# An earlier weight load and an earlier subtraction at the hand-over between two expert layers

## The chip, the cores and the metric

The kernel runs on one core of one Trainium2 chip. The metric is the device time of one launch in microseconds (us). The engines are called as the profile calls them: PE (TensorE, matmuls), PEld (its weight loads), DVE (VectorE), ACT (ScalarE), POOL (GpSimd) and SP (the queue that issues most transfers). "SPq" and "POOLq" are the instruction queues of SP and POOL.

## The reference, cut to what matters

Three layers run one after the other over 7168 tokens of 192 values: a windowed sum with per-token weights, a mixture of 8 experts with two choices per token, and a second mixture with one choice per token. The change lies where the second mixture ends its routing and begins its expert work:

```python
def _moe2_ref(x, expert_emb, tau, w1, w2):
    xn = x / (np.linalg.norm(x, axis=-1, keepdims=True) + 1e-06)
    en = expert_emb / (np.linalg.norm(expert_emb, axis=-1, keepdims=True) + 1e-06)
    logits = xn @ en.T / tau
    expert_idx = np.argmax(logits, axis=1)
    logits_shift = logits - logits.max(-1, keepdims=True)
    probs = np.exp(logits_shift)
    probs /= probs.sum(-1, keepdims=True) + 1e-09
    gate_w = probs[np.arange(N), expert_idx]
    for e in range(E):
        mask = expert_idx == e
        h = np.maximum(x[mask] @ w1[e], 0.0)
        out[mask] = gate_w[mask, None] * (h @ w2[e])
```

## The kernel before, in words

**Tokens and blocks.** Each mixture (`m` = 0, then 1) sorts its tokens by expert into blocks of 256 slots. `positions(m)` on DVE computes each token's slot, turns the slots into one-hot rows (7 groups for m = 1, line 1256), ACT scales half of them by row codes (`hot_rows`, line 1028), and PE multiplies them (line 772) to obtain the list of token rows per slot. DVE then reads that list (`gather_rows`), and the expert work starts.

**Expert work.** `mixture(m)` exists once per engine. For each block `g`, PE computes two products in eight chunks `c` (lines 808 to 824). At chunk `c == TURN_AT` (2) of block g it transposes the token rows of block g+1 (`turn_slots`, lines 789 and 790), for which they must have been gathered: `pe.wait_ge(gathered[m], g * 32 + 64)`. PE takes its instructions in order, so a late gather stops everything behind it. POOL issues each gather as two indirect transfers of 128 rows (line 533), one per half block, from `gather_before(g)`, which fetches block g+3. It waits until PE has turned block g+2, since there is one buffer `x_slots`.

**Gates in the second mixture.** The gathered row of `token_rows[1]` has a last column for the token's gate. The gates are not ready when the first blocks of m = 1 are gathered; blocks 0 to 2 are gathered without them (their gates come by small separate gathers, line 541), and SP meanwhile writes the whole gate column into `token_rows[1]` (line 455, 7168 single values). From block 3 on the gather brings the gate, so `gather_before(0)` on POOL waits for that column: `pool.wait_ge(gate_column_in, 16)`.

**Expert weights.** SP loads each expert's weights (`load_expert`, line 381: four transfers of 512, 256, 256 and 768 KB into `raw1` and `raw2`). ACT and DVE split them into two parts (lines 972, 978, 1310 and 1314) during the first block of the expert before; each finished split raises `weights_ready`, after which `raw` may be overwritten. In m = 1, experts 0 and 1 are loaded before the routing; expert 2 and the later ones come in a loop of SP. That loop stands behind the write of the gate column and, before the change, behind the arrival of the fourth gather (block 3): `sp.wait_ge(gathered[1], 4 * 16 * HALVES)`.

**The subtraction.** The softmax of the second mixture needs each score minus the best one. DVE computes it in `below_best` (line 1372), which `positions(1, below_best)` calls behind the copy of the membership table (line 1204) and ahead of its own wait for PE's ranks (PE lines 758 and 759, then DVE line 1209). `step()` lets DVE wait for the instruction that it has just issued.

Of the kernel before, what the change touches and what calls it, by code (L numbers as in the profile page):

```python
# [16 lines left out]
P = 128  # L17
ALU = mybir.AluOpType
# [8 lines left out]
HALVES = BLOCK // P  # L27
# [24 lines left out]
def attention_moe_moe(nc, x, weight_gen, m_gate, m_noise, noise, w1, w2, emb, tau, v1, v2, w2t, out):  # L52
    B, S, D = x.shape
    H, K = weight_gen.shape[2:]
    E, _, F = w1.shape
    G = D // H
    J = S // P
    T = B * J
# [33 lines left out]
    with ExitStack() as ctx:  # L92
        def sb(name, shape, dt=F32, at=ctx):
            return at.enter_context(nc.sbuf_tensor(name, shape, dt))

        def sem(name):
            return ctx.enter_context(nc.semaphore(name))
# [53 lines left out]
        r = {n: sb(n, [P, T, E]) for n in ("noisy", "tie", "pos", "picked")}  # L151
        onehot = [sb(f"onehot{k}", [P, T, E]) for k in range(2)]
        best = [sb(f"best{k}", [P, T]) for k in range(2)]
# [116 lines left out]
        gate_column_in = sem("gate_column_in")  # L270
# [10 lines left out]
        gathered = [sem(f"gathered{m}") for m in range(2)]  # L281
# [93 lines left out]
        def _(sp):  # L375
# [76 lines left out]
            for b in range(B):  # L452
# [1 line left out]
            sp.wait_ge(gathered[1], 3 * 16 * HALVES)  # L454
            sp.dma_start(tile_rows(token_rows[1], 0, T)[:, :, DS:DS + 1], gate[0][:].unsqueeze(2),
                         allow_slow_non_contiguous=True).then_inc(gate_column_in, 16)
            sp.wait_ge(gathered[1], 4 * 16 * HALVES)

            with sp.Fori(2, E) as e:
                sp.wait_ge(weights_ready, e + E)  # L460
# [202 lines left out]
        def _(pe):  # L663
# [33 lines left out]
            def sum_products(g, inner=None):  # L697

                if g >= 2:
                    pe.wait_ge(rows_ready, g - 1)  # L700
                for n, (tap, _) in enumerate(PAIRS):
                    pe.wait_ge(taps_added, g * len(PAIRS) + n + 1)
                    for h in range(2):
                        ins = mm(banks[:, 2 * (g % 2) + h, 0:GHALF], ident[:], prods[g % 2][:, tap, h * GHALF:(h + 1) * GHALF],  # L704
                                 start=n == 0, stop=n == len(PAIRS) - 1)
                    if n == 1 and inner is not None:
                        inner()
                ins.then_inc(sums_done, 1)
# [159 lines left out]
        def _(act):  # L868
# [80 lines left out]
            def mixture(m, behind_first_split=None):  # L949
                def x_hi(g):  # L950

                    hi_a, _, part_b = x_buffers(parity(act, g))
                    act.wait_ge(x_turned[m], g + 1)
                    sc.copy(hi_a, banks[:, 3, 0:BLOCK])
                    sc.copy(part_b[0:DB], banks[0:DB, 3, BLOCK:]).then_inc(x_hi_ready[m], 1)
# [129 lines left out]
        def _(dve):  # L1085
            v = nc.vector
            steps = [0]

            def step(ins):

                steps[0] += 1
                ins.then_inc(dve_step, 1)
                dve.wait_ge(dve_step, steps[0])
# [49 lines left out]
            def pick(k, scores, at=slice(0, T)):  # L1143

                shape = [P, at.stop - at.start, E]
                tie, top = r["tie"][:, at, :], best[k][:, at]
                step(v.tensor_reduce(top, scores[:, at, :], AX.X, ALU.max))
                step(v.tensor_tensor(tie, scores[:, at, :], top.unsqueeze(2).to_broadcast(shape), ALU.is_equal))
                ranks = expert_rank[:].unsqueeze(1).to_broadcast(shape)
                step(v.tensor_tensor(tie, tie, ranks, ALU.mult))  # L1150
                step(v.tensor_reduce(rank[:, at], tie, AX.X, ALU.max))
                step(v.tensor_tensor(onehot[k][:, at, :], ranks, rank[:, at].unsqueeze(2).to_broadcast(shape), ALU.is_equal))
# [214 lines left out]
            scores = logits[:, :, 0:E]  # L1367
            dve.wait_ge(scores_in, 16)
            pick(0, scores)

            def below_best():
                step(v.tensor_tensor(r["noisy"][:], scores, best[0][:].unsqueeze(2).to_broadcast([P, T, E]), ALU.subtract))

            def weigh_best():
                dve.wait_ge(roots_ready, 1)
# [5 lines left out]
            def finish_best():  # L1381
# [2 lines left out]
                step(v.tensor_scalar(gate_sum[:], gate_sum[:], 1e-9, None, ALU.add))  # L1384
                v.reciprocal(gate[0][:], gate_sum[:]).then_inc(gates_ready[1], 1)

            positions(1, below_best)
            dve.wait_ge(x1_in[NG - 1], 16)
            last = slice((NG - 1) * GROUP, T)
            step(v.tensor_tensor(rows[:, last, :], rows[:, last, :], rows[:, last, :], ALU.mult))  # L1390
# [33 lines left out]
```

## Time and profile before

| What | Value |
|---|---|
| median of 3 runs | 1145.79 us (1145.06 to 1146.03) |
| profiled execution, its time | 1145.06 us |
| its span in the trace | 1143.2 us |
| PE busy | 1055.1 us (92% of the span) |
| DVE, ACT, POOL busy | 708.5, 532.3, 626.9 us |
| granted clock of PE, mean | 0.978 of full speed |

The span is the stretch from the first to the last instruction of the profile; the 1.9 us between it and the execution's time lie around it. Times in the rows further down are microseconds from the start of the span. The first mixture's expert work runs to about 776 us, the second's routing to about 819 us, and its expert work from there to the end.

### The profile page before, as it was taken

What the parts mean: (1) busy time and instruction counts of PE and PEld (TensorE: products, weight loads), DVE (VectorE), ACT (ScalarE), POOL (GpSimd) and SP (SyncE); (2) the same over time, 40 slices, a digit from 0 to 9 for tenths busy, and PEclk for the clock granted to TensorE, in tenths of its full rate; (3) what the DMA queues carried; (4) which work ended last, traced back from release to release, by engine and by line L of the source; (5) the groups of instructions that cost most, each with busy time, mean ns of one, the idle gap of its engine ahead of it and who ended that gap; (6) DMA issues with size and microseconds to landing.
All of it is one profiled execution on the core that took longest, in us unless ns stands there. A gap on an engine that the chain in (4) does not pass through costs nothing.

```text
span 1143.2 us, 27409 instructions
## 1 busy us (share of the span) xinstructions
PE 1055.1 (92%) x7707; PEld 990.4 (87%) x7707; DVE 708.5 (62%) x1474; ACT 532.3 (47%) x1471; POOL 626.9 (55%) x761
## 2 busy tenths in 40 slices
PE   1989988999999999999999999992699999999997
PEld 0556437999999999999999999991499999999997
DVE  8999884556565565555645656444846464567663
ACT  2122574445454454544544545443945454456553
POOL 6888103555565555555556555552265555555554
PEclk9999999999999999999999999996799999999999
DMA  9656995325335252252532524337362231133611
GB/s 333 182 160 166 290 72 131 51 39 105 42 50 98 42 105 41 42 106 41 106 45 39 105 41 83 63 39 143 97 94 74 73 105 42 42 101 99 169 36 35
DMA packets 121939, 106.50 MB, mean 93 GB/s; under 512 B 45971, under 2 KB 111818, under 8 KB 121628
## 3 DMA queue, kind: packets, MB, share of 16 engines
q1 hardware_dynamic: 92316, 69.10, 26.0%
q0 software_dynamic: 29568, 36.73, 18.8%
q8 instruction: 27, 0.44, 0.2%
q14 instruction: 28, 0.23, 0.1%
HBM read 70.61 MB, written 35.73 MB: 93 GB/s over the span
## 4 chain that ended last, share of the span: by engine, by line
PE 79%; DMA 6%; DVE 6%; POOL 3%; issue 2%; ACT 2%; DVEq 0%; SPq 0%; POOLq 0%; ACTq 0%
PE banks L822 23%; PE banks L824 11%; PE banks L808 8%; PE banks L814 7%; PE banks L813 7%; PE banks L809 7%; PE banks L810 7%; PE banks L704 3%; DMA x_slots<-token_rows,gather_idx 3%; DVE prods L1123 3%; POOL prods L521 2%; PE banks L789 2%; PE banks L790 2%; ACT hi_rows L1028 1%; ACT wide L1067 1%
## 5 line engine op out<-in xcount | busy, mean ns | idle before, releaser
L1339 DVE SCALAR_TENSOR_TENSOR h_lo<-banks,h_hi 128x256 fp32r<-128x256 f32 x736 | 312.0, 424 | 351.6 <-ACT h_hi L1009 346.6
L1009 ACT ACTIVATE h_hi<-banks 128x256 fp32r<-128x256 f32 x736 | 283.0, 384 | 433.3 <-PE banks L814 430.2
L822 PE MATMUL banks<-w_hl,h_hi 128*128 128x400 f32 (+1 forms) x1472 | 474.9, 358 | 1.2 <-DVE h_lo L1339 1.2
L824 PE MATMUL banks<-w_hl,h_lo 128*128 128x200 f32 (+1 forms) x1472 | 373.7, 254 | 0.0
L824 PEld LDWEIGHTS banks<-w_hl,h_lo 128*128 128x128 f32 x1472 | 280.3, 190 | 0.0
L822 PEld LDWEIGHTS banks<-w_hl,h_hi 128*128 128x128 f32 x1472 | 277.4, 188 | 1.6 <-issue 1.4
L533 POOL DMA_INDIRECT x_slots<-token_rows,gather_idx x188 | 188.6, 1003 | 112.4 <-POOL gather_idx L526 80.0
L576 POOL DMA_INDIRECT token_rows<-y_slots,store_idx x120 | 194.2, 1619 | 85.5 <-POOL store_idx L571 51.7
L808 PE MATMUL banks<-x_hi_a,w_hi 128*128 (+1 forms) x736 | 221.8, 301 | 1.7 <-DVE x_hl_b L1293 1.7
L810 PE MATMUL banks<-x_lo_a,w_hi 128*128 (+1 forms) x736 | 207.3, 282 | 0.0
L814 PE MATMUL banks<-x_hl_b,w_lo 128*128 (+1 forms) x736 | 207.2, 282 | 0.0
L813 PE MATMUL banks<-x_hl_b,w_hi 128*128 (+1 forms) x736 | 207.2, 282 | 0.0
L809 PE MATMUL banks<-x_hi_a,w_lo 128*128 (+1 forms) x736 | 207.0, 281 | 0.0
L808 PEld LDWEIGHTS banks<-x_hi_a,w_hi 128*128 128x128 f32 x736 | 138.4, 188 | 4.6 <-issue 3.2
L809 PEld LDWEIGHTS banks<-x_hi_a,w_lo 128*128 128x128 f32 x736 | 140.6, 191 | 0.0
L814 PEld LDWEIGHTS banks<-x_hl_b,w_lo 128*128 128x128 f32 x736 | 139.5, 190 | 0.0
L813 PEld LDWEIGHTS banks<-x_hl_b,w_hi 128*128 128x128 f32 x736 | 139.1, 189 | 0.0
L810 PEld LDWEIGHTS banks<-x_lo_a,w_hi 128*128 128x128 f32 x736 | 138.6, 188 | 0.0
L704 PE MATMUL banks<-prods,ident 128*128 128x384 f32 x168 | 67.3, 532 | 34.8 <-POOL prods L521 34.8
L529 POOL COPY gate_ring<-x_slots 128x2 f32 (+1 forms) x89 | 16.8, 189 | 143.8 <-PE banks L790 143.0
L578 POOL DMA_INDIRECT out_rows<-y_slots,store_idx x64 | 66.3, 1037 | 45.3 <-issue 42.0
L1123 DVE TENSOR_TENSOR prods<-x_halo,banks 128x3072 f32<-128x3072 f32 (+1 forms) x28 | 81.3, 2947 | 3.0 <-ACT banks L892 1.8
(194 smaller groups left out, 1133.9 us busy)
## 6 DMA issues: line engine op xcount, KB each, us to landing
raw<-in_moe_w SPq DMA_DIRECT2D x17, 768.0 KB
token_rows<-stage SPq DMA_DIRECT2D x28, 384.0 KB, 4.7
raw<-in_moe_w SPq DMA_DIRECT2D x17, 512.0 KB
raw<-in_moe_w SPq DMA_DIRECT2D x34, 256.0 KB
wide<-in_moe_w_turned SPq DMA_DIRECT2D x8, 768.0 KB, 12.2
token_rows<-zeros SPq DMA_DIRECT2D x14, 402.0 KB, 6.2
x_halo<-in_x SPq DMA_DIRECT2D x2, 2688.0 KB, 15.4
wide<-token_rows SPq DMA_DIRECT2D x14, 384.0 KB, 7.1
```

What stands on the lines that cost most here:

```text
L533: gp.indirect_dma_start(x_slots[:, i, 0:ROWS[m]], None, token_rows[m], bass.IndirectOffsetOnAxis(gather_idx[:, i:i + 1], 0)).then_inc(gath ...
L576: ins = gp.indirect_dma_start(token_rows[1], at, y_slots[:, u, i, :], None, compute_op=ALU.add)
L808: mm(to, w1_hi[u][:, 0, f], hi_a, start=True, stop=False)
L809: mm(to, w1_lo[u][:, 0, f], hi_a, start=False, stop=False)
L810: mm(to, w1_hi[u][:, 0, f], lo_a, start=False, stop=False)
L813: mm(to, w1_hi[u][:, 1, f], part_b, start=False, stop=False)
L814: mm(to, w1_lo[u][:, 1, f], part_b, start=False, stop=True).then_inc(h_done[m], 1)
L822: mm(y[:, i, 0:2 * WIDTH[m]], h_hi[:, c % HBUFS, t], w2_hl[u][:, c, :, 0:WIDTH[m]], start=c == 0, stop=False)
L824: ins = mm(y[:, i, 0:WIDTH[m]], h_lo[:, c % HBUFS, t], w2_hl[u][:, c, 0, 0:WIDTH[m]], start=False, stop=c == FC - 1)
L1009: sc.activation(h_hi[:, c % HBUFS, :], banks[:, c % HBANKS, 0:BLOCK], ACT.Relu).then_inc(h_hi_ready[m], 1)
L1123: v.tensor_tensor(prods[g % 2][:, at:at + n].rearrange("p k (a c) -> p k a c", c=G), x_taps, w_taps, ALU.mult).then_inc(done, 1)
L1339: v.scalar_tensor_tensor(h_lo[:, c % HBUFS, :], banks[:, c % HBANKS, 0:BLOCK], 0.0, h_hi[:, c % HBUFS, :].bitcast(F32), ALU.max, ALU.subtr ...
```

## The change

Two edits. SP's loop over the experts 2 to 7 of the second mixture waits for the gate column to have been written, and no longer for the gather of block 3 to have arrived. DVE subtracts the best score ahead of the membership copy, and no longer between that copy and the wait for the ranks; `positions(1)` is called without a function for that place.

```diff
             sp.wait_ge(gathered[1], 3 * 16 * HALVES)
             sp.dma_start(tile_rows(token_rows[1], 0, T)[:, :, DS:DS + 1], gate[0][:].unsqueeze(2),
                          allow_slow_non_contiguous=True).then_inc(gate_column_in, 16)
-            sp.wait_ge(gathered[1], 4 * 16 * HALVES)
+            sp.wait_ge(gate_column_in, 16)
 
             with sp.Fori(2, E) as e:
                 sp.wait_ge(weights_ready, e + E)
                 load_expert(v1, v2, e)
...
             pick(0, scores)
-
-            def below_best():
-                step(v.tensor_tensor(r["noisy"][:], scores, best[0][:].unsqueeze(2).to_broadcast([P, T, E]), ALU.subtract))
+            step(v.tensor_tensor(r["noisy"][:], scores, best[0][:].unsqueeze(2).to_broadcast([P, T, E]), ALU.subtract))
...
-            positions(1, below_best)
+            positions(1)
```

## Rows read from the trace of the kernel before

**Rows 1.** The page, the chain that ended last, shares by engine.

```profile
PE 79%; DMA 6%; DVE 6%; POOL 3%; issue 2%; ACT 2%; DVEq 0%; SPq 0%; POOLq 0%; ACTq 0%
```

**Rows 2.** Timeline of DVE: start, duration, line, operation, idle before and its releaser.

```profile
793.27 0.62 DVE L1152 TENSOR_TENSOR onehot<-expert_rank,rank 128x448 f32<-128x448 f32 x1
793.93 0.39 DVE L1204 CAST member<-onehot 128x448 bf16<-128x448 f32 x1
794.24 0.61 DVE L1372 TENSOR_TENSOR noisy<-logits,best 128x448 f32<-128x448 f32 x1
795.42 0.62 DVE L1209 COPY counts<-banks 128x448 f32<-128x448 f32 x1 [0.56 <-PE banks L759]
...
802.36 0.46 DVE L1256 TENSOR_TENSOR hots_hi<-column_no,slot_hl 128x576 bf16<-128x576 bf16 x1
...
808.19 0.45 DVE L1256 TENSOR_TENSOR hots_hi<-column_no,slot_hl 128x576 bf16<-128x576 bf16 x1
...
830.03 0.56 DVE L1314 TENSOR_TENSOR w_hl<-raw,w_hl 128x384 fp32r<-128x384 f32 x1
```

**Rows 3.** Timeline of ACT.

```profile
802.92 6.71 ACT L1028 ACTIVATE hi_rows<-hots_hi,row_code_i 128x288 bf16<-128x288 bf16 x14
...
871.30 0.61 ACT L972 CAST w_hi<-raw 128x512 fp32r<-128x512 f32 x1
```

**Rows 4.** The chain that ended last, from 828 us on: start, duration, what.

```profile
827.26 10.81 DMA token_rows<-gate
```

**Rows 5.** Timeline of SP: the first two weight loads of its loop.

```profile
843.34 2.31 SPq L381 DMA_DIRECT2D raw<-in_moe_w  x4
...
881.19 2.62 SPq L381 DMA_DIRECT2D raw<-in_moe_w  x4
```

**Rows 6.** Timeline of PE: turns of gathered rows ahead of which it stood idle.

```profile
177.25 0.30 PE L789 MATMUL banks<-ident,x_slots 128*128 128x128 f32 x1 [4.04 <-DMA x_slots<-token_rows,gather_idx]
...
843.06 0.33 PE L789 MATMUL banks<-ident,x_slots 128*128 128x128 f32 x1 [0.71 <-DMA x_slots<-token_rows,gather_idx]
...
853.54 0.33 PE L789 MATMUL banks<-ident,x_slots 128*128 128x128 f32 x1 [0.50 <-DMA x_slots<-token_rows,gather_idx]
```

**Rows 7.** Timeline of POOL: issues of indirect transfers, and one gate copy.

```profile
840.38 0.95 POOL L533 DMA_INDIRECT x_slots<-token_rows,gather_idx  x1 [0.30 <-issue]
...
845.22 0.99 POOL L578 DMA_INDIRECT out_rows<-y_slots,store_idx  x1 [0.30 <-issue]
...
847.14 0.19 POOL L529 COPY gate_ring<-x_slots 128x2 f32 x1 [0.49 <-POOL gate_ring L546]
...
849.64 0.97 POOL L533 DMA_INDIRECT x_slots<-token_rows,gather_idx  x1 [0.30 <-issue]
...
886.42 0.98 POOL L533 DMA_INDIRECT x_slots<-token_rows,gather_idx  x1 [0.31 <-issue]
```

**Rows 8.** DMA queues, 840 to 842.75 us: packets, MB, share of 16 engines.

```profile
q0 software_dynamic: 96, 0.21, 26.7%
```

**Rows 9.** DMA queues, 844.25 to 847 us.

```profile
q1 hardware_dynamic: 208, 0.77, 91.1%
q0 software_dynamic: 2, 0.01, 1.5%
```

**Rows 10.** DMA queues, 847 to 849.5 us.

```profile
q0 software_dynamic: 52, 0.11, 18.5%
```

**Rows 11.** DMA queues, 886.5 to 889 us.

```profile
q1 hardware_dynamic: 812, 0.65, 104.7%
q0 software_dynamic: 1, 0.00, 0.6%
```

**Rows 12.** DMA queues, 889 to 892 us.

```profile
q0 software_dynamic: 143, 0.30, 31.6%
```

**Rows 13.** Windows: length, busy PE, PEld, DVE, ACT, POOL, granted clock, DMA, GB/s.

```profile
178.00:180.00 2.00, 2.00 (x6) 0.57 (x4) 0.84 (x2) 1.12 (x3) 1.13 (x3) 0.50 0.02 2
180.00:182.00 2.00, 2.00 (x14) 2.00 (x15) 0.35 (x1) 0.77 (x2) 1.09 (x2) 0.75 0.50 66
```

## The prediction

> **What bounds the kernel now.** I read the page first: the chain that ended last is PE for 79% [rows 1]. In the expert work of the second mixture PE runs without gaps, so that a microsecond by which PE stands longer there is a microsecond of the kernel. I then asked for the chain, the waits and the timelines around the place of each edit. The reader should see three things there.
>
> First, the routing. The chain runs from the scores over DVE and ACT to PE. DVE makes the one-hot groups and ACT scales each of them as it comes.
>
> Second, the gate column. Its write takes 10.81 us, from 827.26 to 838.07 [rows 4], and it is on the chain: POOL may gather block 3 only behind it. The second half of that gather is issued from 840.38 to 841.33 [rows 7], PE turns the block at 843.06, and has stood idle for 0.71 us by then [rows 6]. There is thus no slack at all in the gather of block 3.
>
> Third, the weight load of expert 2. SP issues it at 843.34 [rows 5], right behind the arrival of that gather. It is not this load's own data that anybody waits for, neither before nor after the change, as shown below. What matters is which gathers it shares the DMA engines with.
>
> **The subtraction (DVE).** Nothing is added or removed, one instruction of 0.61 us moves. Where it stands now it is free: DVE ends it at 794.85 and stays idle for another 0.56 us until PE's ranks release the copy at 795.42 [rows 2]. Where it goes, it lies ahead of the membership copy, and PE's ranks, the counts and everything behind them wait for that copy. Its price there is its pitch with the step's wait, read at its neighbour of the same shape: 793.27 to 793.93, 0.66 us, call it 0.65. The idle gap behind the copy grows from 0.56 to what it takes without the subtraction, and pays nothing back.
>
> Could ACT hide it? ACT squares the rows of the first eight groups before it turns to the one-hot groups, and starts those at 802.92; the first group has been ready since 802.36 + 0.46 = 802.82. At the last of the seven groups DVE is ready at 808.19 + 0.45 = 808.64, and ACT, whose 14 instructions end at 802.92 + 6.71 = 809.63, that is 0.96 a group, starts it at about 808.67 [rows 2, 3]. So ACT lags by 0.10 us at first and by 0.03 at the end: of 0.65 us it hides 0.03. The term is **+0.6 us** (bounds 0.55 and 0.66). Behind it the list of rows, the gathers, the gates and the column all shift by as much.
>
> **SP's wait.** The new wait ends when the column has landed, 838.07 + 0.6 = 838.7. The other wait of the loop, for the split of expert 1, ends with the last DVE part at 830.03 + 0.56 = 830.6 [rows 2], and is no cover. From the arrival of what released it to its first issue SP took about 0.3 us before (843.06 to 843.34). The load is then issued from 839.0, 4.9 us before its shifted old place of 843.9. In SP's queue only the later loads of the loop stand behind it, and each of those waits for a split of its own.
>
> What does the earlier load bring? Nothing: ACT reads expert 2's `raw` first at 871.30 [rows 3], some 20 us after the load is through. It has a cost, since POOL issues the gather of block 3 at the same moment: its second half from 841.0 to 841.9, 2 to 3 us behind the start of a load of 1792 KB.
>
> **How late does a gather come that shares the engines with such a load?** Alone, the whole gather is 96 packets, all served by 842.75 [rows 8], 1.4 us behind the end of its second issue; PE moves 1.7 us behind that end. With a load there are three places to read:
>
> (a) The gather of block 4. Its second issue ends at 850.61 and PE moves at 853.54 [rows 6, 7]: 2.9 us instead of 1.7, so 1.2 us late. It meets only the tail of its load, having been issued 7.3 us behind the load's start.
>
> (b) The second load, issued at 881.19 [rows 5]. The gather beside it has its second issue done at 887.40 [rows 7]. From 886.5 to 889 the software queue q0, which serves POOL's transfers, moves 1 packet while q1 moves 812 [rows 11]; then 143 packets pass from 889 to 892 [rows 12]. If they end at 892, that is 4.6 us behind the issue instead of 1.4: 3.2 us late. PE does not stand idle for it there, since it comes to that block later; behind 853.54 no such stop is left in the expert work.
>
> (c) The nearest in position: POOL's two stores of block 0. The second is issued from 845.22 to 846.21 [rows 7], 1.9 to 2.9 us behind the load of 843.34, just where the second half of block 3's gather will stand. In 844.25 to 847 q0 moves 2 packets beside 208 of q1 [rows 9], 52 in the next 2.5 us [rows 10]. So the first store is through at about 849 and the second at about 851, some 7.7 us behind the load's start. A gather in its place is through at 839.0 + 7.7 = 846.7, instead of 842.75 + 0.6 = 843.4: 3.3 us late.
>
> I take **+3.2 us**, by (b) and (c), because they lie in the body of a load, as the new gather does. The bounds: nothing, if the gather's packets slip in before the load has filled the engines (its first half is issued 1.3 us ahead of its second, hardly a microsecond behind the load); and at the far end (b) taken whole, 892 less 881.19 = 10.8 us behind the load's start, which is 849.8 and 6.4 us late.
>
> The same two rows may be held against a rule. Beside (c) q1 moves 208 packets and q0 2, though both queues hold work for at least part of that window. The Trainium skill, page "DMA: Bandwidth & Descriptors", section "Queues, rings and completion order", says that each DMA engine takes turns between its queues, a packet at a time. By that rule the gather would hardly suffer, and the sum would be that of the third rival below; rows 9 and 11 do not look like taking turns.
>
> **What goes away.** The gather of block 4 no longer meets the load: it is issued at about 849 to 851.2, when a load issued at 839.0 has been through since about 848 (that of 843.34 is through near 852). POOL is not late for it, for its own work holds it until 847.14 + 0.6 = 847.7 [rows 7], and PE has turned block 3 by 843.7 + 0.6 + 3.2 = 847.5. PE's 0.50 us ahead of block 4's turn [rows 6] therefore vanishes, the more surely as PE itself arrives 3.8 us later: **-0.5 us** (bounds -0.5 and 0).
>
> **The sum.** 0.6 + 3.2 - 0.5 = +3.3 us. The profiled execution took 1145.06 us (span 1143.2 and 1.9 around it) and would take 1148.4; the median of the runs shown is 0.73 us above it, so 1145.79 + 3.3 = **1149.1 us**.
>
> **The rivals.** No change that can be told is one within 0.2% of the time, 2.3 us.
>
> Rival 1, the clock falls as well. PE would stand idle for 0.71 + 3.2 = 3.9 us. Once before it stood for 4.04 us at such a turn [rows 6], and the granted clock was then 0.50 (1.2 GHz) from 178 to 180, and 0.75 on average from 180 to 182 [rows 13]; nearly 3.5 us at half speed in all, which costs half of that, 1.7 us. Against it: the gap is shorter, and the stops of 0.7 us left the clock alone. It gives 1149.1 + 1.7 = 1150.8 us. Chance 0.2. With the far bound of the gather (+6.4 and the clock) it would be 1154; chance 0.05.
>
> Rival 2, not slower: the gather of block 3 gets its packets served nearly at once, because load and gather start together and the load's queue is not yet deep. Then only 0.6 - 0.5 = +0.1 us stay, 1145.9 us. The case turns at a delay of 2.2 us, below which the sum stays under 2.3 us. For it speaks that no row shows a gather so early in a load; against it rows 9, where 2 packets passed. Chance 0.07.
>
> Rival 3, taking turns: the delay is the 1.2 us of (a). The rows give a size for it too: q1's packets are 0.77 MB / 208 = 3.7 KB, moved at 0.77 MB / 2.75 us = 280 GB/s [rows 9]; 96 of them, one ahead of each of the gather's, are 1.3 us. Then 0.6 + 1.2 - 0.5 = +1.3, 1147.1 us, no change that can be told. Chance 0.2.
>
> Rival 4, faster by over 2.3 us: it would need a stop that the earlier load removes, and I find only the 0.5 us. Chance 0.03.
>
> **How the numbers follow.** The forecast has 0.45, rival 1 with the far bound 0.25: slower 0.70. Rivals 2 and 3 make 0.27 for within 0.2%, leaving 0.03 for faster. The range runs from 1146.2, which leaves out rival 2 and nearly nothing of rival 3, to 1152.0, which takes in rival 1 with a delay of 4.4 us and leaves out the far bound. The forecast's own range (delay 2.2 to 4.4 us) is 1148.1 to 1150.3.
>
> **What the profile after would show.** SP issues its load near 839 instead of 843.3. DVE: the subtraction at 793.9, the membership copy at 794.6, counts at 796.1, and PE's first one-hot product 0.6 us later than before. PE: the idle time ahead of the turn at chunk 2 of block 2 is 3.9 us and not 0.71, and the 0.50 us one block on is gone. q0 moves almost nothing from 841 to 843. The span ends 3.3 us later. The prediction is wrong if PE's idle time there stays under 2 us, if the clock falls behind it, or if ACT turns out to set the pace of the one-hot groups and hides the 0.6 us.

## The result, and the profile after

The changed kernel took 1152.26 us (median of 6 runs, 1150.19 to 1154.53) beside 1144.09 us (1142.07 to 1146.03) for the kernel before: a ratio of 1.0070 with a 95% interval of 1.0054 to 1.0087, or 8.2 us slower. The sign was forecast, the size was not: 3.3 us were forecast, and the time lies 0.3 us above the range. The runs of before beside it were also 1.7 us lower in the median than the three shown ahead of the prediction. Measured twice more, on two chips, the same kernel gave 1.0037 (1.0023 to 1.0051) and 1.0061 (1.0040 to 1.0081).

The profiled execution has a span of 1148.8 us beside 1143.2. First the timeline of DVE after, which answers to [rows 2]:

```profile
791.41 0.62 DVE L1152 TENSOR_TENSOR onehot<-expert_rank,rank 128x448 f32<-128x448 f32 x1
792.07 0.63 DVE L1370 TENSOR_TENSOR noisy<-logits,best 128x448 f32<-128x448 f32 x1
792.73 0.40 DVE L1204 CAST member<-onehot 128x448 bf16<-128x448 f32 x1
794.14 0.62 DVE L1209 COPY counts<-banks 128x448 f32<-128x448 f32 x1 [1.02 <-PE banks L759]
```

The subtraction takes 0.66 us with its wait, and the idle gap behind the membership copy grows from 0.56 to 1.02 us. From the one-hot of the best expert to the counts it is 2.15 us before and 2.73 after. Next the place of the other edit: the chain that ended last, then SP's, POOL's and PE's timelines after. They answer to [rows 4 to 7].

```profile
826.35 11.54 DMA token_rows<-gate
837.95 0.19 POOL gather_idx L526
...
840.21 7.50 DMA x_slots<-token_rows,gather_idx
```

```profile
838.22 2.33 SPq L381 DMA_DIRECT2D raw<-in_moe_w  x4
```

```profile
838.93 0.97 POOL L533 DMA_INDIRECT x_slots<-token_rows,gather_idx  x1 [0.80 <-POOL gather_idx L526]
840.21 0.95 POOL L533 DMA_INDIRECT x_slots<-token_rows,gather_idx  x1 [0.30 <-issue]
```

```profile
847.76 0.47 PE L789 MATMUL banks<-ident,x_slots 128*128 128x128 f32 x1 [6.71 <-DMA x_slots<-token_rows,gather_idx]
```

```profile
859.24 0.27 PE L789 MATMUL banks<-ident,x_slots 128*128 128x128 f32 x1
```

SP issues the load 0.7 us ahead of the gather's first half. The second half's issue ends at 841.16, and PE moves 6.60 us later; before, it was 843.06 less 841.33, 1.73 us [rows 6, 7]. The gather is therefore **4.87 us later** than alone, and PE stands idle for 6.71 us and not 0.71. One block on, at 859.24, there is no stop any more where before there was one of 0.50 us.

The DMA queues after, from 840 to 842, 842 to 844, 844 to 845, 845 to 847 and 847 to 848 us (packets, MB, share of 16 engines):

```profile
q1 hardware_dynamic: 169, 0.61, 95.2%
q0 software_dynamic: 4, 0.02, 8.2%
```

```profile
q1 hardware_dynamic: 122, 0.30, 69.8%
q0 software_dynamic: 43, 0.08, 21.9%
```

```profile
q1 hardware_dynamic: 223, 0.19, 107.6%
q0 software_dynamic: 1, 0.00, 0.1%
```

```profile
q1 hardware_dynamic: 705, 0.54, 91.1%
q0 software_dynamic: 48, 0.11, 17.1%
```

```profile
q0 software_dynamic: 96, 0.19, 53.6%
q1 hardware_dynamic: 90, 0.06, 19.5%
```

Alone the gather needs 96 packets of q0 and had them within 2.75 us [rows 8]. Here the same 96 take from 841 to 847: 48 of them, as many as one half of the gather, by 845, and 48 more, beside 705 of q1, by 847. The 96 behind them are as many as POOL's two stores need, which it had issued by 846.02. The load is through at about 847.5. Last the windows of PE (columns as in [rows 13]):

```profile
847.00:848.00 1.00, 0.24 (x1) 0.23 (x2) 0.00 (x0) 0.00 (x0) 0.00 (x0) 0.50 0.73 248
848.00:849.00 1.00, 1.00 (x6) 0.94 (x5) 0.00 (x0) 0.00 (x0) 0.00 (x0) 0.50 0.00 0
...
851.00:852.00 1.00, 1.00 (x8) 1.00 (x7) 0.48 (x2) 0.38 (x1) 0.69 (x2) 0.79 0.00 0
852.00:853.00 1.00, 1.00 (x10) 1.00 (x9) 0.28 (x2) 0.48 (x2) 1.00 (x2) 1.00 0.39 103
```

The clock has fallen to half (1.2 GHz) during the stop, and PE works at half speed until about 851.5. From the turn in block 2 to that in block 3 it is 859.24 - 847.76 = 11.48 us; before it was 10.48 with the stop of 0.50 in it.

**Where the time went, counted from the load of the scores** (SP line 448, 784.59 before, 782.55 after, which takes out a start that differs by chance). To the issue of the column +1.13 us: 0.6 of the subtraction, and 0.55 that the second gather of block 2 took longer (4.10 us instead of 3.55). The column itself +0.73 (11.54 instead of 10.81). Column to gather issue 0. The gather +4.87. Turn to turn +1.00, the half clock less the 0.50 us stop. From there to the end -0.10. The sum is +7.63 us. Less the 2.04 us of the earlier start it is the 5.6 us between the spans.

### The profile page after: what moved, and what is told of

Its sections match the earlier page's. It is cut to its first block, busy times and chain, and to the rows that moved or that the text cites. A ratio compares the mean times of both kernels' runs of the same rounds, so it can differ in the third digit from the quotient of the medians.

```text
span 1148.8 us, 27408 instructions
## 1 busy us (share of the span) xinstructions
PE 1056.2 (92%) x7707; PEld 990.7 (86%) x7707; DVE 708.8 (62%) x1474; ACT 531.4 (46%) x1471; POOL 624.3 (54%) x761
## 4 chain that ended last, share of the span: by engine, by line
PE 79%; DVE 9%; DMA 5%; POOL 3%; issue 2%; ACT 1%; DVEq 0%; POOLq 0%; ACTq 0%; SPq 0%
PE banks L822 23%; PE banks L824 11%; PE banks L808 9%; PE banks L814 7%; PE banks L813 7%; PE banks L809 7%; PE banks L810 7%; DVE prods L1123 4%; DMA x_slots<-token_rows,gather_idx 2%; POOL prods L521 2%; PE banks L789 2%; PE banks L790 2%; PE banks L704 2%; ACT hi_rows L1028 1%; DMA token_rows<-gate 1%
```

## The experiments

Fifteen runs of kernels, in four groups on four chips. Ratios are to the kernel before on the same chip.

### One edit at a time

`sp_alone` has SP's edit only, `sub_alone` DVE's only.

```diff
-            sp.wait_ge(gathered[1], 4 * 16 * HALVES)
+            sp.wait_ge(gate_column_in, 16)
```

> Only SP's wait is changed; the subtraction stays behind the membership copy. The changed kernel was 8 us slower than before. Theory: the gather of block 3 is starved by the load of expert 2 that now starts with it, and PE's clock falls in the long stop. Then this run is 6.5 to 7.5 us slower than before, PE stands idle for 5.5 to 6.5 us ahead of the turn in block 2, and the clock falls behind it. Rival: both edits count about equally, because the shift of the routing moves PE's warm-up against the clock; then this run is only 3 to 4 us slower.

Measured 1153.34 us, ratio 1.0044 (1.0028 to 1.0060), 5.1 us at the before of 1148.92 (4.4 us between the medians). PE's stop was 6.44 us, from the end of the second issue (843.32) to the turn 5.79 us, that is 4.1 us later than alone. The column took 12.44 us in this profile. The clock fell. The stop is there as expected, but the time is not: 6.5 to 7.5 us were expected by the theory, 3 to 4 by the rival, and 5.1 lies between them.

> Only the subtraction is moved; SP waits for the fourth gather as before. Theory: +0.6 us, the stops of PE at the turns stay 0.7 and 0.5 us. Rival (both edits count): +3 to +4 us, with the gate column or PE's first blocks slower than before.

Measured 1148.29 us, ratio 1.0006 (0.9994 to 1.0018): 0.7 us, in keeping with the +0.6 us but not apart from nothing. Its stop at the turn was 1.79 us, not 0.7, since the column took 11.92 us. The two edits add up to 1.0050, which lies between the three measurements of both. SP's edit is the one that costs. What could not be expected stands in PE's timeline and windows of this run:

```profile
845.81 0.33 PE L789 MATMUL banks<-ident,x_slots 128*128 128x128 f32 x1 [1.79 <-DMA x_slots<-token_rows,gather_idx]
```

```profile
844.00:846.00 2.00, 0.21 (x3) 0.19 (x3) 0.77 (x2) 0.60 (x3) 1.27 (x4) 1.00 0.20 56
846.00:848.00 2.00, 2.00 (x10) 1.96 (x9) 0.00 (x0) 0.00 (x0) 1.08 (x2) 0.52 0.36 66
848.00:850.00 2.00, 2.00 (x13) 2.00 (x12) 0.63 (x2) 0.38 (x1) 1.45 (x4) 0.63 1.04 331
```

A stop of 1.79 us was followed by half clock for 3.4 us.

### The clock, taken out

`sp_filled` has SP's edit, and in block 2 PE runs idle matmuls ahead of its wait:

```diff
                         if c == TURN_AT:
+                            for _ in range(fill):     # 28 in block 2 of m = 1, else 0
+                                mm(banks[:, 3, :], ones[:], ones[:].unsqueeze(1).to_broadcast([P, 4, P]), start=True, stop=True)
                             pe.wait_ge(gathered[m], g * 32 + 64)
```

> SP's wait changed as in the changed kernel, subtraction as before; in addition PE runs 28 idle matmuls of 128x512 into the free bank 3 in block 2 ahead of its wait for the gather of block 3 (about 6 us of PE time at full clock), so that it is busy while the gather is late. No result changes. Theory: the clock stays at 1.0, and this run is 1 to 2 us faster than the one with SP's wait alone. Rival (the clock fell for another reason, or costs nothing): same time as that run within 0.5 us.

Measured 1151.20 us, ratio 1.0019 (1.0008 to 1.0031), 2.1 us below `sp_alone` on the same chip by the medians and 2.9 by the ratios, whose intervals overlap a little. PE's turn and the window from 844 to 852 us of `sp_alone`, then of `sp_filled`:

```profile
849.11 0.48 PE L789 MATMUL banks<-ident,x_slots 128*128 128x128 f32 x1 [6.44 <-DMA x_slots<-token_rows,gather_idx]
```

```profile
844.00:852.00 8.00, 2.89 (x13) 2.83 (x14) 0.00 (x0) 0.00 (x0) 3.71 (x9) 0.59 0.75 189
```

```profile
850.08 0.33 PE L789 MATMUL banks<-ident,x_slots 128*128 128x128 f32 x1 [0.49 <-DMA x_slots<-token_rows,gather_idx]
```

```profile
844.00:852.00 8.00, 7.51 (x41) 4.27 (x40) 0.77 (x2) 0.22 (x2) 4.56 (x10) 1.00 0.91 244
```

The mean granted clock there is 1.00 instead of 0.59, and turn to turn it is 859.90 - 850.08 = 9.82 us instead of 860.35 - 849.11 = 11.24. So the fallen clock costs about 1.4 us by the profiles and 2.1 by the medians, on top of the delay of the gather. That delay was 3.7 us in this profile (850.08 less 844.66, less 1.73), the smallest of the five that have SP's edit.

### What starves the gather

`load_behind_issue` starts the load just behind the issue of the gather:

```diff
-            sp.wait_ge(gathered[1], 4 * 16 * HALVES)
+            sp.wait_ge(gates_taken[1], 1)
```

> Kernel before, but SP's loop waits for gates_taken[1] >= 1, which POOL raises about 0.2 us behind the issue of the gather of block 3 (841.5 in the trace before); the load starts 1.5 us earlier than before and 3.5 us later than in the changed kernel, with the gather already in its queue. Theory (what is queued first is served first): the gather is not late, PE's stop there stays 0.7 us, the stop one block on shrinks, time 0 to 0.5 us below before. Rival (any load beside a gather delays it): PE's stop grows to 2 us or more, and the time by 1.5 us or more.

Measured 1148.55 us, ratio 0.9998 (0.9984 to 1.0012). The load was issued at 843.23, 0.5 us behind the end of the gather's issue (842.69), and PE moved at 844.41, 1.72 us behind that end: no delay at all. Its stop was 1.85 us, longer than expected, from a column of 12.08 us and not from the load; the clock fell to 0.50 behind it. A gather whose issue ended 0.5 us ahead of the load's start was not held up; one whose issue began 0.7 us behind that start was 3.7 to 4.9 us late in five profiles.

`early_w1` and `early_w2` split the load. In the first the three transfers of `raw1` (1024 KB, rows of 4 KB) go out behind the column and that of `raw2` (768 KB, rows of 768 bytes) behind the gather; in the second the other way round.

```diff
-            sp.wait_ge(gathered[1], 4 * 16 * HALVES)
+            sp.wait_ge(gate_column_in, 16)
+            sp.wait_ge(weights_ready, 2 + E)
+            load_parts(v1, v2, 2, EARLY)      # (0, 1, 2) or (3,)
+            sp.wait_ge(gathered[1], 4 * 16 * HALVES)
+            load_parts(v1, v2, 2, LATE)       # (3,) or (0, 1, 2)
```

> Kernel before, but of the four transfers of expert 2's load the three of raw1 (1024 KB in rows of 4 KB) go out behind the gate column, as in the changed kernel, and the one of raw2 (768 KB in rows of 768 bytes) only behind the arrival of the gather of block 3. With the whole load early that gather arrives 6.6 us behind the end of its issue, alone 1.7. Theory (the gather waits for what the load's queue holds, by bytes): the early part is through about 4.3 us behind its start, that is 1.5 us behind the end of the gather's issue, and the gather comes 0.5 to 2 us late; time +0.5 to +2 us. Rival (the small packets of raw2 are what starves it, and rows of 4 KB do not): gather 0 to 0.5 us late, time as before.

> The other way round: raw2 (768 KB in rows of 768 bytes) goes out early, the three transfers of raw1 behind the gather's arrival. Theory (by bytes): as the run with raw1 early or a little less, gather 0.5 to 2 us late. Rival (small packets starve it): gather 3 to 5 us late, time +3 us or more. A second rival (queues take turns packet by packet): small packets delay least, gather under 0.3 us late.

The gather's arrival is read from the transfer that SP issues behind it. In the kernel before that is 2.01 us behind the end of the gather's issue (843.34 less 841.33). SP's timeline of `early_w1`, then of `early_w2`, the early and the late part:

```profile
838.43 1.50 SPq L389 DMA_DIRECT2D raw<-in_moe_w  x3
...
846.12 0.39 SPq L389 DMA_DIRECT2D raw<-in_moe_w  x1
```

```profile
837.77 0.38 SPq L389 DMA_DIRECT2D raw<-in_moe_w  x1
...
843.25 1.51 SPq L389 DMA_DIRECT2D raw<-in_moe_w  x3
```

The gathers' issues ended at 841.67 and 841.02. So `early_w1` has 4.45 us and is 2.4 us late, `early_w2` 2.23 us and is 0.2 us late. The DMA queues show why. `early_w2` from 840 to 842 us, then `early_w1` from 842 to 844:

```profile
q1 hardware_dynamic: 882, 0.67, 98.5%
q0 software_dynamic: 24, 0.09, 13.0%
```

```profile
q1 hardware_dynamic: 96, 0.31, 78.0%
q0 software_dynamic: 24, 0.08, 19.5%
```

`raw2` alone is through by 842, one microsecond behind the gather's issue, and the gather follows it at once. `raw1` is through near 844.5, and the gather is in by 845.5. In the first profile after, the whole load is through near 847.5 and the gather with it. So the delay grows with the bytes ahead, as the theory had it; it put `raw2` too high, at 0.5 to 2 us. But the gather does not always wait for the load's end. The DMA queues of `sp_filled` from 850.1 to 851 us, behind PE's turn at 850.08, and of the kernel before from 846.5 to 848, beside the load of 843.34:

```profile
q0 software_dynamic: 89, 0.19, 60.6%
q1 hardware_dynamic: 129, 0.09, 32.4%
```

```profile
q1 hardware_dynamic: 101, 0.35, 68.3%
q0 software_dynamic: 48, 0.10, 28.8%
```

In the first PE has the whole gather and the load still has 129 packets to go; in `sp_alone` it is the same, with about 70. In the second a store of 48 packets passes in the middle of a load. Of the rivals, that small packets starve the gather more is refuted (0.2 us instead of 3 to 5). The second, taking turns packet by packet, forecast under 0.3 us for `raw2`, which is what came; fewer bytes explain that as well, and these runs do not part the two. The Trainium skill (page "DMA: Bandwidth & Descriptors", section "Queues, rings and completion order") has each DMA engine take turns a packet at a time and puts such a packet at about 9 to 17 descriptors. Taking turns by the profile's own packets does not fit: q0, with most of its 96 waiting, passes 24 beside 96 of q1. But those are single rows of the load (0.44 MB / 551 is 800 bytes), so the counts do not decide against the rule of the Trainium skill, and how the engines choose between the queues stays open.

The times: `early_w1` 1146.72 us, ratio 0.9996 (0.9986 to 1.0006); `early_w2` 1146.38 us, 0.9988 (0.9979 to 0.9997). For `early_w1` 0.5 to 2 us more were expected and none came. Its PE had stopped for 1.46 and 1.16 us in block 1 already, and asked for the gather that much later: its stop at the turn was only 0.69 us.

### What the kernel before loses by itself

> The kernel before once more, for its profile on this chip. The runs so far showed the write of the gate column at 10.8, 11.5, 11.9, 11.9, 12.1 and 12.4 us, and with it stops of PE of 0.7 to 1.8 us where the gather was not starved, the longer ones followed by 3.4 us at half clock. Theory (the column's duration varies by itself): this profile too may show a column over 11.5 us, a stop over 1.3 us and the clock falling. Rival (the longer column comes from the edits): 10.8 us, a stop of 0.7 us and the clock at 1.0.

1146.42 us. Neither: the column took about 11.2 us, there was no stop at the turn at all, and PE reached it at 845.22, later than before (843.06), having stopped in block 1. ACT's and PE's timelines of this run:

```profile
834.58 0.38 ACT L1009 ACTIVATE h_hi<-banks 128x256 fp32r<-128x256 f32 x1 [3.94 <-remote]
```

```profile
835.48 0.69 PE L822 MATMUL banks<-w_hl,h_hi 128*128 128x384 f32 x1 [2.78 <-DVE h_lo L1339]
```

ACT stands for 3.94 us, with a releaser from outside the engines, DVE and PE wait behind it, and the clock falls. The first profile of before has no such stop.

> The changed kernel beside the others on one chip. The sum of the two edits alone measured 0.44% + 0.06%. Theory: where the kernel before already loses its clock at this place, the changed one loses less against it than in its first measurement: ratio 1.004 to 1.006 and a stop of 6 to 7 us. Rival: 1.007 again whatever the kernel before does.

1150.13 us, ratio 1.0037 (1.0023 to 1.0051). The ratio is just below the 1.004 to 1.006 of the theory, whose stop of 6 to 7 us did not come. The gather was 4.80 us late (848.04 less 841.51, less 1.73) as in the first profile, but PE had already stopped for 0.20 and 1.84 us in block 1. Its stop at the turn was 2.80 us, and the clock stayed at 1.00:

```profile
848.04 0.33 PE L789 MATMUL banks<-ident,x_slots 128*128 128x128 f32 x1 [2.80 <-DMA x_slots<-token_rows,gather_idx]
```

```profile
848.00:850.00 2.00, 1.96 (x16) 1.96 (x16) 0.00 (x0) 0.03 (x1) 0.32 (x2) 1.00 0.06 18
```

`column_small` writes 896 of the 7168 gates and leaves the other rows' gates zero, so that its outputs are not the reference's:

```diff
-            sp.dma_start(tile_rows(token_rows[1], 0, T)[:, :, DS:DS + 1], gate[0][:].unsqueeze(2),
+            sp.dma_start(tile_rows(token_rows[1], 0, T)[:, 0:7, DS:DS + 1], gate[0][:, 0:7].unsqueeze(2),
```

> Kernel before, but SP writes the gate column for the first 7 of the 56 tiles only, 896 values instead of 7168; the outputs of later blocks are then scaled with zero gates for the rows left out, the work and its order are the same. Theory (the column is what sets the gather of block 3, and its 7168 packets also hold up the small transfers beside it, the gathers of gates and the loading of code): no stop of PE at the turn in block 2, no stops of ACT or PE of over 1 us in block 1, no fall of the clock; 1.5 to 4 us faster than before. Rival (the stops in block 1 come from elsewhere): they stay, and only 0.7 to 1.8 us are won.

Measured 1146.09 us, ratio 0.9992 (0.9980 to 1.0003). The stops in block 1 stayed (ACT 3.51 us released from outside, PE 1.37 and 1.94 us), and at the turn there was none: POOL had waited for PE and no longer for the column. So the theory that the column's packets make those stops falls, as far as one profile tells; the rival is right about them, and even the 0.7 us at the turn were hardly won.

> The changed kernel a third time, beside the kernel before on one chip. Theory (the change costs the gather's 4 to 5 us at the turn in block 2, less what the kernel before loses there by itself, which differs from execution to execution): ratio 1.003 to 1.006, and the 1.007 of the first measurement was its upper edge. Rival (the change costs 8 us, and the second measurement was low): 1.006 or more.

1155.37 us, ratio 1.0061 (1.0040 to 1.0081): on the edge between theory and rival, with the 1.0070 inside its interval. The gather was 4.92 us late. Its stop at the turn was 2.78 us, behind which the clock stayed at 1.00; it had fallen already in block 1. This profile is of one of the two quickest executions, 1150.90 us, 4.5 below the median: these two have a mean granted clock of 0.978, the other four, 1155.15 to 1157.33 us, one of 0.971 to 0.975. So the profile does not show where most of the 7 us of this timing went; the clocks suggest that part of it is lost at half clock, but not where.

> The kernel before on the same chip, for its profile alone. Theory: of its time ahead of the turn in block 2 PE loses 0.7 to 4 us, either in a stop at the turn or in stops of block 1 released by DVE or ACT, with or without a fall of the clock. Rival: as in the first profile, 0.7 us and nothing else.

1150.33 us. As the theory had it, and more than its 4 us: ACT stood for 3.60 us, PE for 0.61 and 2.03 us in block 1, the clock fell, and PE reached the turn without a stop, 64.4 us behind the load of the scores. The first profile of before needs 58.5 us for that and `before_again` 62.1; the three of after need 65.2, 63.7 and 65.4.

### Versions meant to be faster

`before_filled` puts 8 idle matmuls ahead of the wait in the kernel before.

> Kernel before with 8 idle matmuls of 128x512 (1.7 us) into the free bank 3 in block 2 ahead of PE's wait for the gather of block 3. No result changes. Theory: the clock stays at 1.0 there; where the kernel before loses it the run is 1 to 1.7 us faster, elsewhere up to 1 us slower (1.7 less the stop of 0.7). Rival: the clock falls all the same.

1146.58 us, ratio 0.9994 (0.9980 to 1.0008); no difference. `four_gates` takes the column off the path of block 3: the gates of four blocks are gathered by themselves, and only the gather of block 4 waits for the column.

```diff
-                    if m == 1 and isinstance(g, int) and g == 0:
+                    first = m == 1 and isinstance(g, int) and g < 2
+                    if first and g == 1:
                         pool.wait_ge(gate_column_in, 16)
-                    else:
+                    if not first:
                         take_gates(g + 2)
...
+                    for g in (1, 2):
+                        gather_before(g)
+                        store_block(g, g % 2)
-                with pool.Fori(0, pool.snap(full // 2)) as pair:
+                with pool.Fori(m, pool.snap(full // 2)) as pair:
```

> Kernel before, but the gates of block 3 are gathered by themselves too, as those of blocks 0 to 2, so that the gather of block 3 no longer waits for the gate column (the first that does is that of block 4). Theory (column, stop and clock are the whole loss at this place): no stop ahead of the turn in block 2, the clock stays, the load starts behind the column or the gather and meets the gather of block 4, which has room; 1 to 3.5 us faster than before, by what the kernel before loses on this chip. Rival: the gather of block 3 or 4 is then late behind the column's or the load's packets, stops of 1 us or more stay, same time as before.

1149.75 us, ratio 1.0027 (1.0015 to 1.0039): slower. No stop stands at the turn in block 2, but PE stopped for 1.31, 1.00 and 2.30 us by DVE and by "issue", and the clock fell at 846.9. Why this version has more such stops was not followed up.

`load_behind_5th` lets SP's loop wait for `5 * 16 * HALVES`.

> Kernel before, with SP's loop behind the fifth gather (block 4), which then no longer meets the load; that of block 5 does, and has 3 us or more of room. Theory: PE's stop of 0.5 us ahead of the turn in block 3 goes, where it is there; 0 to 0.5 us faster than before. Rival: the gather of block 5 comes too late instead, +1 us or more.

1146.63 us, ratio 0.9988 (0.9977 to 0.9999). That is 1.4 us by the ratio, more than the 0.5 that the stop in block 3 can give, and 0.4 us between the medians, with an interval that all but touches 1.

> Kernel before with SP's loop behind the fifth gather and 8 idle matmuls (1.7 us) ahead of PE's wait in block 2: the two edits that gained or cost nothing by themselves. Theory: 0.5 to 2 us faster than before (0.5 for the stop in block 3, up to 1.7 where the clock would have fallen). Rival: the idle matmuls cost as much as they save, same time as with SP's edit alone (0.12% faster).

1150.03 us, ratio 1.0012 (0.9999 to 1.0025). The gain does not come again with the idle matmuls added. No version is shown to beat the kernel before by more than 0.2%.

## Why the prediction was right and wrong

**The subtraction (+0.6 us).** Right in the profile: 0.58 us longer from one-hot to counts, ACT now waiting 0.45 us for the first group. By itself it measured 0.06% +/- 0.12%, which does not contradict it and does not show it.

**SP's wait, and no use for the earlier load.** Right: load at 838.22, read by ACT from 876.96 on.

**What goes away (-0.5 us).** Right: no stop ahead of block 3's turn.

**How late the gather comes (+3.2 us): the term that was mis-sized.** It is 4.8 to 4.9 us in the three profiles of the changed kernel, and 4.1 and 3.7 in the two that have SP's edit alone. The load and the gather came as forecast, the gather's second issue ending 2.9 us behind the load's start. What failed is the place (c) as a measure: it put the gather 7.7 us behind the load's start, as it did POOL's second store, and PE had it only 8.4 to 9.6 us behind. The place (b), too, says less than was read from it: rows 12 count 143 packets where the gather has 96, so that 892 is not its end alone but that of a store as well. The far bound, 6.4 us, had been built from that row, but was taken to be a tail. The load of 843.34 has its last packets at about 852.5 and not 852. With "the load's end less the gather's own end when alone" the term would have been 839.0 + 9.2 - 843.4 = 4.8 us. That is close to the changed kernel's, but too much for `sp_alone` and `sp_filled`, in which PE had the gather before the load's end.

**Rival 3, taking turns (1.2 to 1.3 us).** As a size it failed. Its sum took one row of the load for each of the gather's packets, and between 845 and 847 us 705 passed beside 48. Turns of larger packets were not priced and are not tested here.

**The clock, rival 1 (+1.7 us, chance 0.2).** The sum put this term at nothing, and that is the second step that failed. The fall came in the first profile and in that of `sp_alone`; it cost 1.5 us in the first (1.00 from turn to turn and the 0.50 of the stop that went), and `sp_filled` measured 2.1 us for it. With 4.9 us of delay PE's stop is 6 to 7 us, and the sentence that the stops of 0.7 us left the clock alone carried little: `sub_alone` has it falling behind 1.79 us and `load_behind_issue` behind 1.85. In `after_again` and `after_third` it stayed behind 2.8 us; that stops in block 1 had gone before may be the reason, which no run tests.

**The sum.** 0.6 + 4.9 - 0.5 + 1.7 = +6.7 us with the gather as measured and the clock at rival 1's price, beside 8.2, 7.1 and 3.6 us between the medians of the three timings. The rest of the profiles' difference is 1.3 us by which a gather and the column took longer, and those two durations change between runs of one kernel too: the column 10.8 to 12.4 us over all kernels. Rival 1 with the far bound, chance 0.05, adds up to the measured 8.2 us, but by luck: its 6.4 us of delay did not come.

The spread of the three timings has a partner in the profiles: before the turn, the kernel before loses between 0.7 and about 6 us by itself, and what is lost there already is not lost again to the late gather. That this makes the spread is argued from single profiles, not shown by timing, and it does not fit the third timing, whose profiles lie only 1.0 us apart at the turn and whose medians lie 7.1 apart. What makes ACT stand 3.5 to 3.9 us in block 1 is open; the column does not. The forecast also took one quiet profile for the kernel before.

## What to carry to other kernels

A wait that seems to hold back a transfer for nothing may be what keeps it out of another's way: look at which small transfer is about to be issued, and put the large one behind its issue, which cost nothing here (0.9998, 0.9984 to 1.0012), and not ahead of it, which made the small one 3.7 to 4.9 us late beside a load of about 9 us. Price the collision near the large load's end, and read a place of the same kind of transfer before taking another kind for it. Then ask whether the stop that results is long enough for PE's clock to fall, and whether the profile of before is a typical one or merely the quiet one.

## What was not expected of the hardware

- POOL's indirect gather of 0.2 MB, its second half's issue ending 2.9 us behind the start of a load of 1792 KB on SP's queue, was 3.7 to 4.9 us late in five profiles, and in three of them PE had it before the load's last packets; with its issue ending 0.5 us ahead of the load, it was not late at all.
- The granted clock fell to 0.50 for 3.4 us behind a stop of PE of only 1.79 us, and stayed at 1.00 behind ones of 2.80 and 2.78 us that had others some 10 us before them.
- One write of 7168 single values took 10.8 to 12.4 us from run to run, and with 896 of them the kernel was no faster than its interval of 0.1% can tell.
